# Down-projection by seven block products: sums of activations in place, weight parts made once in the expert tiles

## The reference, cut to what matters

```python
def _attn_ref(q, k, v): ...                     # decayed linear attention, 4 x 8 heads x 768 x 64
def _moe_ref(x, modality_id, w_gate, modality_bias, w1, w2):
    ...
    for e in range(E):                          # 8 experts, one per token
        h = np.maximum(x[mask] @ w1[e], 0.0)
        out[mask] = gate_w[mask, None] * (h @ w2[e])
    return out
def _moe2_ref(x, w_in, w_out):                  # x 3072 x 512, w_in 512 x 2048, w_out 2048 x 512
    h = x @ w_in
    g = h * (1.0 / (1.0 + np.exp(-1.702 * h)))
    return (g @ w_out).astype(np.float32)
```

## Time and profile before

| | us |
|---|---|
| three timed runs, median | 967.67 |
| lowest and highest of them | 962.67, 969.55 |
| profiled execution, its own time | 969.25 |
| its span, first to last instruction | 967.7 |
| TensorE busy in the span | 948.6 |
| mean granted TensorE clock | 0.993 |

### The profile page before, as it was taken

The page is one execution under the profiler, slowest core; times in us unless marked ns, Lnnn a source line. Parts: engine busy times, 40 slices in busy tenths (PEclk is TensorE's granted clock), DMA queues, the critical chain, the costliest instruction groups (busy, mean ns, idle before and its releaser), DMA issues.

```text
span 967.7 us, 16741 instructions
## 1 busy us (share of the span) xinstructions
PE 948.6 (98%) x5941; PEld 777.3 (80%) x5942; DVE 486.0 (50%) x759; ACT 410.0 (42%) x657; POOL 247.3 (26%) x279
## 2 busy tenths in 40 slices
PE   7999999999999999999999999999999999999997
PEld 5777877888888888888788888888888888888886
DVE  3487584222222222234756884555687545666453
ACT  2335522222222222233666654356665445565442
POOL 4435416655333765300120001032000200000011
PEclk8999998999999999999999999999999999999999
DMA  7778586656344657211452224464123444223342
GB/s 255 248 284 316 182 187 196 218 196 209 119 131 143 237 196 250 66 46 68 127 188 66 86 89 136 147 211 137 66 88 87 153 141 163 88 87 87 98 134 73
DMA packets 51721, 145.19 MB, mean 150 GB/s; under 512 B 6204, under 2 KB 6372, under 8 KB 47540
## 3 DMA queue, kind: packets, MB, share of 16 engines
q1 hardware_dynamic: 30160, 85.50, 27.5%
q0 software_dynamic: 11504, 40.74, 12.9%
q10 hardware_dynamic: 9972, 17.89, 5.2%
HBM read 100.81 MB, written 34.90 MB: 140 GB/s over the span
## 4 chain that ended last, share of the span: by engine, by line
PE 94%; DMA 2%; issue 1%; DVE 1%; ACT 1%; POOL 0%; SPq 0%; POOLq 0%; ACTq 0%; DVEq 0%
PE bank L1738 26%; PE bank L1740 26%; PE bank L1739 26%; PE bank L1777 2%; PE bank L1648 2%; PE bank L1622 2%; DMA qk_in<-qk 2%; PE bank L1657 1%; PE bank L1600 1%; PE bank L1638 1%; PE bank L1609 1%; PE bank L1857 1%; PE bank L1668 1%; PE bank L1682 1%; PE bank L1689 0%
## 5 line engine op out<-in xcount | busy, mean ns | idle before, releaser
L1740 PE MATMUL bank<-w_hi,act_lo 128*128 128x512 f32 x384 | 150.3, 391 | 0.0
L1738 PE MATMUL bank<-w_hi,act_hi 128*128 128x512 f32 x384 | 150.1, 391 | 0.0
L1739 PE MATMUL bank<-comb_lo,act_hi 128*128 128x512 f32 x384 | 150.0, 391 | 0.0
L1738 PE MATMUL bank<-mix_hi,w_hi 128*128 128x512 f32 x336 | 131.8, 392 | 1.7 <-ACT h_sum L835 0.8
L1740 PE MATMUL bank<-mix_hi,comb_lo 128*128 128x512 f32 x336 | 131.6, 392 | 0.0
L1739 PE MATMUL bank<-mix_lo,w_hi 128*128 128x512 f32 x336 | 131.0, 390 | 0.0
L835 ACT ACTIVATE w_hi<-comb 128x1024 fp32r<-128x1024 f32 x96 | 96.0, 1002 | 76.0 <-PE bank L1740 73.2
L784 POOL DMA_INDIRECT out<-f_out,token_idx x24 | 26.1, 1088 | 385.6 <-ACT f_out L835 303.2
L1162 DVE TENSOR_TENSOR hT_lo<-bank,hT_hi 128x512 fp32r<-128x512 f32 x52 | 35.8, 691 | 119.4 <-ACT hT_hi L835 119.4
L1497 DVE TENSOR_TENSOR comb_lo<-comb,w_hi 128x1024 fp32r<-128x1024 f32 x48 | 58.7, 1224 | 72.6 <-ACT w_hi L835 71.8
L1503 DVE TENSOR_TENSOR h_sum<-bank,h_sum 128x512 f32<-128x512 f32 x72 | 49.5, 689 | 78.9 <-PE bank L1740 78.7
(11 more groups left out here) (238 smaller groups left out, 1641.5 us busy)
## 6 DMA issues: line engine op xcount, KB each, us to landing
comb<-w_comb SPq DMA_DIRECT2D x24, 1024.0 KB, 5.1
comb<-w_out SPq DMA_DIRECT2D x48, 512.0 KB, 3.5
qk_in<-qk SPq DMA_DIRECT2D x24, 512.0 KB, 4.0
raw<-w SPq DMA_DIRECT2D x24, 512.0 KB, 6.3
weights<-raw POOLq DMA_DIRECT2D x16, 512.0 KB, 4.6
w_comb<-mix_in POOLq DMA_DIRECT2D x8, 1024.0 KB, 4.3
y_slots<-y_out ACTq DMA_DIRECT2D x26, 256.5 KB, 4.3
v_in<-v SPq DMA_DIRECT2D x24, 256.0 KB, 5.5
```

The lines of the kernel that those rows point to most:

```text
L1738: mm(dst, hi, w_hi, start=first, stop=False, skip_group_check=skip)
L1739: mm(dst, hi, w_lo, start=False, stop=False, skip_group_check=skip)
L1740: return mm(dst, lo, w_hi, start=False, stop=last, skip_group_check=skip)
```

## The change

The down-projection becomes seven block products as well. Its blocks are the two token sides of 512, the two halves of the hidden chunks (0 to 7, 8 to 15) and two halves of 256 output columns. The products run in the order P1, P5, P6, P2, P7, P3, P4 (`DOWN_ORDER`). Each goes over eight chunks in four steps of two; a step is 2 chunks x 4 token tiles x 3 matmuls of 256 columns.

The activation sums T1 to T4 are made by VectorE in place in `act_f` (`mix_t1` to `mix_t4`, 128x1024 but for T1), just ahead of the product that uses them. A step's operand is split as 128x1024 into one of two buffers (`act_high` on ScalarE, `act_low` on VectorE). Three products share one set of PSUM banks; partial results are copied to SBUF (`keep_x`, `keep_y`) and added when the output tile is written (`add_c22`, `add_pair`, `take_out`). The last two steps of P4 run tile by tile.

All weight sums, of `w_in` and now of `w_out` too, are made in the expert tiles 3 to 18, one set of four blocks per tile: ScalarE loads it, VectorE adds (`sum_quads`), ScalarE makes the high part (`part_high`), VectorE the low part (`part_low`), and ScalarE stores both parts to `w_parts` in three DMAs (`store_parts`). GpSimd no longer takes part. In stage 3 SP loads finished high and low parts into a ring of four buffers: two pieces for a pair of the up-projection, two for a product of the down-projection, each of these in two DMAs of 512 KB with rows of 1 KB. `early_hi`, `late_hi`, `out_hi` and their low counterparts are gone. GpSimd stores the second half of the output tiles ahead of the first.

The diff, cut to its core (added lines only; the code that goes is in the print above):

```diff
+RING, RING_COLS = 4, 1024
+assert RING_COLS >= max(LATE_COLS, EARLY_W)
+ACT_BUFS, ROW_BUFS, FIRST_BUFS = 2, 4, 6
+STEP = 2
+STEPS = PAIRS_F // STEP
+DOWN_ORDER = (P1, P5, P6, P2, P7, P3, P4)
+HALF_PRODUCTS = 2
+CHUNKS_IN_RING = PAIRS_F // HALF_PRODUCTS
+assert CHUNKS_IN_RING * QUAD == RING_COLS
+GROUP_PIECES = 2 * PAIRS_F + HALF_PRODUCTS * PRODUCTS
+DOWN_STEPS = STEPS * PRODUCTS - 1
...
+                    cols = slice(0, LATE_COLS) if k % 2 else slice(LATE_COLS, PART_COLS)
+                    sp.dma_start(ring[buf][:, :, 0:cols.stop - cols.start].bitcast(F32), w_parts[k // 2, :, :, cols]).then_inc(
+                        ring_in[buf], DMA_INC)
                 else:
+                    q, half = divmod(k - 2 * PAIRS_F, HALF_PRODUCTS)
+                    first, col = PAIRS_F + CHUNKS_IN_RING * half, part_at(ENTRY[DOWN_ORDER[q]])
+                    for part_ in range(2):
+                        sp.dma_start(ring[buf][:, part_, :].rearrange("p (c d) -> p c d", d=QUAD).bitcast(F32),
+                                     w_parts[first:first + CHUNKS_IN_RING, :, part_, col:col + QUAD].rearrange(
+                                         "c p d -> p c d")).then_inc(ring_in[buf], DMA_INC)
+            sp.wait_ge(parts_stored, DMA_INC * MIX_STORES * MIXES)
...
+            def store_parts(n, buf):
+                act.wait_ge(part_hi_done, n * 2 + 2)
+                act.wait_ge(part_lo_done, n * 2 + 2)
+                to = lambda part_, lo, hi: w_parts[bass.ds(n, 1), :, part_, lo:hi].rearrange("a p f -> p (a f)")
+                act.dma_start(to(0, 0, PART_COLS), part_hi[:, :].bitcast(F32)).then_inc(parts_stored, DMA_INC)
+                act.dma_start(to(1, 0, LATE_COLS), mix_in_lo[buf][:, 0:LATE_COLS].bitcast(F32)).then_inc(parts_stored, DMA_INC)
+                act.dma_start(to(1, LATE_COLS, PART_COLS), mix_in_lo[buf][:, EARLY_AT:].bitcast(F32)).then_inc(parts_stored, DMA_INC)
+            def part_high(n, buf):
+                act.wait_ge(quads_mixed, n + 1)
+                copy(part_hi[:, 0:LATE_COLS], mix_in[buf][:, 0:LATE_COLS]).then_inc(part_hi_done, 1)
+                copy(part_hi[:, LATE_COLS:], mix_in[buf][:, EARLY_AT:]).then_inc(part_hi_done, 1)
+            def mixing_step(i, n, buf, first=False, last=False):
+                store_y(i - 2, True)
+                if not first:
+                    store_parts(n - 1, 1 - buf)
+                take_hidden(i)
+                x_hi(i + 1)
+                hidden_hi(i)
+                if not first:
+                    act.wait_ge(parts_stored, n * (DMA_INC * MIX_STORES))
+                if not last:
+                    load_quads(n + 1, 1 - buf)
+                part_high(n, buf)
...
+            def act_high(g, q, c):
+                product = DOWN_ORDER[q]
+                t = down_at(g, q, c)
+                if t >= ACT_BUFS:
+                    act.wait_ge(act_used, buffer_used(t - ACT_BUFS))
...
+                if product == P5:
+                    act.wait_ge(act_mixed, t1_count(g, STEP * c + STEP - 1))
+                if product == P6:
+                    act.wait_ge(act_mixed, t2_count(g, c))
+                if product in (P2, P3):
                     act.wait_ge(act_done, 4 * PAIRS_F * (g + 1))
+                if product == P7:
+                    act.wait_ge(act_mixed, t3_count(g, c))
+                if product == P4:
+                    act.wait_ge(act_mixed, t4_count(g, c))
+                copy(act_hi[:, t % ACT_BUFS], operand(product, c)).then_inc(act_hi_done, 1)
...
+                act_high(g, 0, 1)
                 sigmoid_last(g, PAIRS_F - 1)
+                next_high(g + 1, P1, 0)
+                act_high(g, 0, 2)
+                next_high(g + 1, P5, 1)
+                act_high(g, 0, 3)
+                next_high(g + 1, P6, 1)
+                for q in range(1, PRODUCTS):
+                    product = DOWN_ORDER[q]
+                    for c in range(STEPS):
+                        act_high(g, q, c)
+                        if product == P5 and c == 1:
+                            keep_x(g, q - 1, p1_kept)
+                        if product == P6:
+                            if c == 0:
+                                next_high(g + 1, P3, 3)
+                            if c == 1:
+                                keep_y(g, q - 1, kept[:, 1])
+                                next_high(g + 1, P7, 0)
+                            if c == 2:
+                                next_high(g + 1, P2, 2)
+                        if product == P2 and c == 1:
+                            keep_x(g, q - 1, kept[:, 0])
+                        if product == P3 and c == 0:
+                            next_high(g + 1, P4, 1)
...
+            def sum_quads(n, nth, buf):
+                e = lambda at_: mix_in[buf][:, at_ * QUAD:(at_ + 1) * QUAD]
+                dve.wait_ge(quads_in[buf], nth * DMA_INC + DMA_INC)
+                tt(e(S1_AT), e(A21_AT), e(A22_AT), ALU.add).then_inc(quads_step, 1)
+                tt(e(S3_AT), e(A11_AT), e(A21_AT), ALU.subtract)
+                dve.wait_ge(quads_step, n * 2 + 1)
+                tt(e(S2_AT), e(S1_AT), e(A11_AT), ALU.subtract).then_inc(quads_step, 1)
+                dve.wait_ge(quads_step, n * 2 + 2)
+                tt(e(S4_AT), e(A12_AT), e(S2_AT), ALU.subtract).then_inc(quads_mixed, 1)
+            def part_low(n, buf):
+                for nth, (cols, hi) in enumerate(((slice(0, LATE_COLS), part_hi[:, 0:LATE_COLS]),
+                                                  (slice(EARLY_AT, COMB), part_hi[:, LATE_COLS:]))):
+                    dve.wait_ge(part_hi_done, n * 2 + (nth + 1))
+                    tt(mix_in_lo[buf][:, cols], mix_in[buf][:, cols], hi.bitcast(F32), ALU.subtract).then_inc(part_lo_done, 1)
+            def mixing_step(i, n, nth, buf):
+                sum_quads(n, nth, buf)
                 expert_step(i, True)
+                part_low(n, buf)
...
+                act_low(g, 0, 1)
+                mix_t1(g, PAIRS_F - 1)
+                next_low(g + 1, P1, 0)
+                act_low(g, 0, 2)
+                next_low(g + 1, P5, 1)
+                next_mix(g + 1, 2, 1, 3, 1)
+                act_low(g, 0, 3)
+                next_low(g + 1, P6, 1)
+                for q in range(1, PRODUCTS):
+                    product = DOWN_ORDER[q]
+                    for c in range(STEPS):
+                        if product == P7:
+                            for ahead in (0, 1) if c == 0 else (c + 1,):
+                                if ahead < STEPS:
+                                    mix_t3(g, ahead)
+                        act_low(g, q, c)
+                        if product == P5:
+                            mix_t2(g, c)
+                        if product == P2:
+                            mix_t4(g, c)
+                        if product == P6:
+                            if c == 0:
+                                next_low(g + 1, P3, 3)
+                            if c == 1:
+                                next_mix(g + 1, 3, 0, 1, 0)
+                                next_low(g + 1, P7, 0)
+                            if c == 2:
+                                next_low(g + 1, P2, 2)
+                        if product == P7 and c == STEPS - 1:
+                            next_mix(g + 1, 4, 1, 2, 1)
+                        if product == P3:
+                            if c == 0:
+                                next_low(g + 1, P4, 1)
+                            if c == 1:
+                                add_c22(g, q - 1)
+                            if c == 2:
+                                add_pair(g, q - 2, 0, down_Z, p1_kept)
+                        if product == P4 and c == 1:
+                            add_pair(g, q - 1, HT, down_Y, kept[:, 0])
...
+            def ff_down(g, q):
+                product = DOWN_ORDER[q]
+                if product == P6:
+                    pe.wait_ge(down_kept, kept_p1(g))
+                if product == P7:
+                    pe.wait_ge(down_kept, kept_u1(g))
+                if product == P3:
+                    pe.wait_ge(down_kept, kept_p5(g))
+                if product == P4:
+                    pe.wait_ge(out_added, added_c22(g))
+                tail = STEPS // 2 if product == P4 else STEPS
+                for c in range(tail):
+                    down_ready(g, q, c)
+                    for j in range(HT):
+                        if product == P1 and c == 0:
+                            if j < 2 and g + 1 < GROUPS:
+                                pe.wait_ge(fT_copied, GT * (g + 2))
+                            elif j < 2:
+                                pe.wait_ge(out_copied[j], HT // 2 * g)
+                            if j == 2:
+                                pe.wait_ge(h_ready, 3 * (PAIRS_F * g + PAIRS_F - 1) + 1)
+                            if j == 3:
+                                pe.wait_ge(act_done, 4 * PAIRS_F * (g + 1))
+                        last = down_products(g, q, c, j)
```

(30 more changed lines are left out.)

511 lines of the change are left out of this document (242 added, 269 removed).

## The result

The changed kernel takes 992.40 us in the median of four runs (988.29 to 995.11), the kernel before 965.61 in the four beside them: a ratio of 1.0271, 95% interval 1.0215 to 1.0328. It is slower. I had forecast 964.5 with a range from 948 to 983. The profiled execution took 995.11 us against 969.25, 25.9 more.

The account below looks back on a forecast made before the run. TensorE, busy 98% of the span, was taken as the bound: tail time is matmul count times spacing, plus stalls. 969.25 - 32.8 + 23.0 - 1 + 6 = 964.5 us, range 948 to 983.

Parts of the forecast that it names:

- -1: Start of the up-projection: first weight splits no longer stand ahead of the h_sum TensorE awaits; -1 us (0 to -2).
- I take 113.7: Down-projection matmuls: 256 columns cost half of 227.3 ns, so 229.1 us instead of 261.9, -32.8 us.
- half-clock row: Profile row of 512-column matmuls at 1.2 GHz, 426.7 ns each; implies 14 of 227.3 ns at full clock are something else.
- transposes: Profile row used to support 113.7: four in 0.60 us, 110 ns each, carrying no 14 ns.
- 44-column row: Profile row of 24 narrow matmuls, 111.5 ns each, limited by the weight load; lower bound of 224.8 us for the down-projection.
- rival with the fixed cost: Down-projection matmuls keep a fixed 14 ns each, 120.7 ns at 256 columns; time 976, chance 0.19.
- +23.0: Down-projection: TensorE waits for operands at its start, P6's third step, P7's first step and P4's tail; bounds 8 to 31.
- my 2.7: P4's tail: the bare rounding and subtraction chain stalls TensorE 2.72 us in each of three groups.
- +6: Expert tiles: some four tiles wait for store landings of 8 to 11 us, 0.5 to 3 us each; +6 us.
- my loop: Expert tiles: store landing plus 4.5 us of roundings, subtraction and issues; fits a 12.3 us tile for landings up to 7.8.
- store loop sets their pace: Rival: landings past 7.8 us cost every expert tile; at 10 us +33 in place of +6, 991.5, chance 0.17.

Follow-up runs that it names:

- small_stores: Changed kernel, storing only 128 of 1792 columns per half for 15 of 16 weight blocks, the ring always reading block 0: 986.14 us, ratio 1.0222.
- tail_one_step: Changed kernel with only the last step of the seventh product run tile by tile, not the last two: 976.78 us, ratio 1.0107.
- before_moved_64: Kernel before the change, with 64 matmuls in a never-taken branch ahead of TensorE's loop over the tiles: 964.70 us in one execution.
- after_moved_64: Changed kernel with 64 matmuls in a never-taken branch ahead of TensorE's loop over the tiles: 991.19 us in one execution.
- fine steps: Changed kernel with down-projection steps of one chunk and four buffers, sums for the seventh product spread earlier, tail of two chunks: 980.27 us, ratio 1.0122.
- fine_c: Changed kernel with both the one-chunk down-projection steps and the expert-tile order of expert_c: 959.68 us, ratio 0.9947.
- expert_c: Changed kernel, reordered expert tiles: high half stored once rounded, other stores and next load later, sums just before the hidden layer's low half: 976.61 us, ratio 1.0113.

## Why the prediction was wrong

- **Which stage bounds what** was read rightly: the tail's time is matmuls times spacing plus stalls, and the splits of the weights were hidden. The up-projections gained 3.3 us where I had -1, since no weight split stands before the first h_sum and the first group's 82.8 became 80.3.
- **"I take 113.7" is the first step that failed.** The 14 ns of a 512-column matmul are a cost per matmul: 120.0 - 106.7 = 13.3 at 256 columns, 227.3 - 213.3 = 14.0 at 512, and nothing at the lower clock (0.213 us). The half-clock row had said it, and I had set it aside for the transposes and for the 44-column row, where the load is the limit. The matmuls gave -20.0 us, not -32.8. The rival with the fixed cost was right here. (The load row's own quotient is 111.3, not 111.5, which changes nothing.)
- **The stalls, +23.0,** came to 27.8 - 1.5 = +26.3. Their places were all four as written: in the first group TensorE idles 1.67 us at the start, 1.27 at P6's third step, 1.38 at P7, 2.61 in the tail. The gaps themselves make 22.1 us, so the term was right in them; what it left out is the lower clock behind them. In the trace of after the clock stayed at 2.4 GHz behind the waits up to 1.67 us and fell to 1.2 behind each tail. That is no rule: in small_stores the 1.67 us at the start of the first two groups were followed by the lower clock (from 550.75 and 721.42 us) and the first tail's 2.61 were not. tail_one_step measured the tail at 4.1 us a group against my 2.7.
- **"+6" for the expert stage is the step that cost most:** it was 22.9. It said that some four tiles would meet landings of 8 to 11 us and pay 0.5 to 3 us each. Four tiles paid most of it, but 5.0, 1.4, 7.5 and 6.8 us. They lay at 174 to 225 and 349 to 368 us, where I had named 190 and 320. Three things were missing. The landings went to 12.7 us. TensorE, idle behind ScalarE's wait, then runs at the lower clock (0.93 over those stretches). And VectorE's two low halves, 0.95 and 1.22 us in my sum, took up to 6.9 together while GpSimd worked, and ScalarE stood 33.7 us for them at the head of its steps, a wait that my loop did not have. Another 5.3 us lie in the hand-over, 2.5 the stop and 2.8 the lower clock behind it; that they came with the change is shown, why is not. The first tiles gave 3.8 back, but that is chance: the transposes that begin at 178.07 before and 174.25 after begin at 173.14 in before_moved_64 and at 179.33 in after_moved_64.
- **The rival "store loop sets their pace"** gave 991.5, and the time came out there by luck, not by its mechanism: it wanted a late store in all tiles, and eight tiles in a row took 12.3 us. The measured time is the fixed cost a matmul, tails at their true price, and four tiles held much longer than I had them.
- **The sum** with the terms as measured is 969.25 - 20.0 + 26.3 - 3.3 + 22.9 = 995.15, the profiled 995.11. It is an account of where the time lies; the test are the runs that undo a term: the order in the expert tiles gives back 15.8 us in the median, fine steps and tail 12.1, and together they give the 959.68 of fine_c.

The Trainium skill (SBUF — State Buffer, "Who interferes with whom") says of a VectorE subtraction with both inputs in SBUF and a GpSimd operation that reads SBUF that the second to start waits until the first is done, and that one with an input in PSUM isn't held. The traces agree on both. hT_lo, which reads PSUM, never took long (min/median/max), though eight of its runs began while a GpSimd tensor_tensor was at work:

```profile
L1252 DVE TENSOR_TENSOR hT_lo<-bank,hT_hi x52: 679/692/693, 135.3 to 471.6; 128x512 fp32r<-128x512 f32 x52
```

But they show more than one operation's length: 5.7 us over two of GpSimd's (2.41 us each) and the DMA issue between them.

## What to carry to other kernels

Price a matmul from two rows that differ in clock or width, and split it in a fixed part and one per column; halving the columns keeps the fixed part. When work is added to a queue that feeds TensorE, write the queue out in order and ask for each wait what stands behind it: a wait that is free on average costs its whole length, and at times the slow clock after it, in the few tiles where it bites. A store should be waited for only where its buffer is needed again, and work that another engine waits for should stand ahead of work that nobody does; in this kernel that order (expert_c) was worth at least as much as storing next to nothing. And a start read from one trace is one draw: small_stores had 17.2 us there and 6.3 in the median.

## What I had not expected of the hardware

- A VectorE subtraction of 64 columns from SBUF, 0.22 us alone, lasted up to 5.6 us while GpSimd worked; cutting VectorE's work to it saved nothing.
- The issue of a DMA takes ScalarE's own time: 0.34 us at the least, but up to 1.38 us for one of the stores. Six DMA issues a tile are work on the engine that the table of busy times doesn't count.
- With 12.3 us tiles TensorE ran at the full clock with 0.98 of the DMA engines busy; traffic alone did not slow it.
- A stop of 2.5 to 3.1 us at a branch, which ends 2.8 to 2.9 us after a packet starts that I take for TensorE's next instructions; that it is the cause was not tested.
